# Attention of an attention, MoE and FFN kernel: two-step periods in a fixed order, the odd copies of transposed probabilities divided

## The reference

```python
batch, n_heads, seq, head_dim = (2, 8, 768, 64)
q_bits = (np.einsum('bhsd,dk->bhsk', q, proj) > 0)      # k_bits likewise
mask = q_bucket[:, :, :, None] == k_bucket[:, :, None, :]
scores = scale * np.matmul(q, k.transpose(0, 1, 3, 2))
scores = np.where(mask, scores, -1000000000.0)
scores = scores - np.max(scores, axis=-1, keepdims=True)
attn = np.exp(scores)
attn = attn / (np.sum(attn, axis=-1, keepdims=True) + 1e-09)
return np.matmul(attn, v)
```

## Time and profile before

| what | us |
|---|---|
| median of three runs | 1029.27 (1027.99 to 1030.33) |
| the profiled execution, its own time | 1037.7 |
| its span, first to last instruction | 1035.6 |
| TensorE busy in the span | 920.9 (89%) |
| VectorE, ScalarE, GpSimd busy | 428.7 (41%), 348.8 (34%), 416.7 (40%) |
| mean granted TensorE clock | 0.953 |

### The profile page before, as it was taken

The page is one execution under the profiler, slowest core; times in us unless marked ns, Lnnn a source line. Parts: engine busy times, 40 slices in busy tenths (PEclk is TensorE's granted clock), DMA queues, the critical chain, the costliest instruction groups (busy, mean ns, idle before and its releaser), DMA issues.

```text
span 1035.6 us, 15081 instructions
## 1 busy us (share of the span) xinstructions
PE 920.9 (89%) x4789; PEld 746.9 (72%) x4790; DVE 428.7 (41%) x756; ACT 348.8 (34%) x616; POOL 416.7 (40%) x247
## 2 busy tenths in 40 slices
PE   3699999999975389969999999999389999999998
PEld 3566666666643368858888888888279999999996
DVE  4567776677535812212222222222354333333222
ACT  1576677666734011111111111111223232323222
POOL 1222110000028585799594857689695001000000
PEclk8899999999998589989999999999789999999999
DMA  7444653356014279744352525245432011000000
GB/s 161 114 123 110 159 137 85 94 138 168 1 76 162 81 254 343 242 151 155 112 165 94 162 81 172 89 154 162 134 130 82 21 51 38 33 0 0 31 1 31
DMA packets 73237, 116.45 MB, mean 112 GB/s; under 512 B 31920, under 2 KB 33968, under 8 KB 73200
## 3 DMA queue, kind: packets, MB, share of 16 engines
q1 hardware_dynamic: 60592, 86.61, 28.0%
q0 software_dynamic: 4400, 14.42, 4.8%
q10 hardware_dynamic: 8208, 14.95, 4.4%
HBM read 73.49 MB, written 23.59 MB: 94 GB/s over the span
## 4 chain that ended last, share of the span: by engine, by line
PE 73%; DVE 7%; POOL 7%; DMA 6%; SPq 2%; issue 2%; ACT 2%; POOLq 0%; ACTq 0%; DVEq 0%
PE psS L726 13%; PE psT L683 12%; PE psS L667 11%; PE psS L741 9%; PE psV L565 6%; PE psT L554 4%; PE psV L741 4%; PE psS L543 4%; POOL W L433 3%; POOL W L431 2%; DMA x_sb<-x_dram,gather_i 2%; DVE W L796 2%; PE psS L692 2%; PE psM L530 2%; DMA staged<-in_moe_w 2%
## 5 line engine op out<-in xcount | busy, mean ns | idle before, releaser
L431 POOL TENSOR_TENSOR W<-staged,ones_col 128x1024 fp32r<-128x1024 f32 x80 | 152.7, 1909 | 167.9 <-DMA staged<-in_moe_w 103.8
L433 POOL TENSOR_TENSOR W<-staged,W 128x1024 fp32r<-128x1024 f32 x80 | 192.8, 2410 | 6.3
L667 PE MATMUL psS<-W,xT_hi 128*128 x448 | 144.4, 403 | 2.0 <-DVE xT_lo L969 2.0
L726 PE MATMUL psS<-x2T_hi,W 128*128 (+1 forms) x512 | 134.0, 343 | 1.6 <-DVE x2T_lo L987 1.6
L683 PE MATMUL psT<-W,hT_hi 128*128 x448 | 124.5, 410 | 9.2 <-POOL W L433 9.2
L802 DVE TENSOR_REDUCE neg_max<-psS 128x1 f32<-128x768 f32 x96 | 91.6, 954 | 48.9 <-PE psS L543 48.0
L1038 ACT ACTIVATE prob<-psS,exp_arg 128x768 f32<-128x768 f32 x96 | 95.5, 994 | 32.8 <-DVE exp_arg L805 32.7
L543 PE MATMUL psS<-W 128*128 128x384 f32 x384 | 93.4, 366 | 10.7 <-DMA W<-k_hi 9.3
L726 PEld LDWEIGHTS psS<-x2T_hi,W 128*128 128x128 f32 x512 | 94.5, 191 | 6.8 <-issue 2.0
L683 PEld LDWEIGHTS psT<-W,hT_hi 128*128 128x128 f32 x448 | 81.2, 191 | 24.7 <-issue 9.4
L1047 ACT ACTIVATE probT<-psT 128x768 f32<-128x768 f32 x96 | 78.1, 813 | 61.0 <-PE psT L554 59.5
(11 more groups left out here) (170 smaller groups left out, 1295.2 us busy)
## 6 DMA issues: line engine op xcount, KB each, us to landing
staged<-in_moe_w SPq DMA_DIRECT2D x64, 512.0 KB, 3.5
xs_dram<-x_sb SPq DMA_DIRECT2D x31, 256.0 KB, 4.8
x_in<-xs_dram ACTq DMA_DIRECT2D x29, 256.0 KB, 2.7
ys_dram<-y_sb ACTq DMA_DIRECT2D x28, 256.0 KB, 2.4
W<-q_hi SPq DMA_DIRECT2D x32, 192.0 KB, 3.4
W<-k_hi SPq DMA_DIRECT2D x32, 192.0 KB, 3.7
staged<-in_moe_w_in SPq DMA_DIRECT2D x8, 512.0 KB, 3.6
staged<-in_moe_w_out SPq DMA_DIRECT2D x8, 512.0 KB, 3.4
```

Source lines behind the costliest of these rows:

```text
L431: nc.gpsimd.tensor_tensor(W[:, at:at + CH], staged[:, n % 2], ones_col[:].to_broadcast([P, CH]), ALU.mult).then_inc(s_whi, 1)
L433: nc.gpsimd.tensor_tensor(W[:, at + BLOCK:at + BLOCK + CH], staged[:, n % 2], W[:, at:at + CH].bitcast(F32), ALU.subtract).then_inc(s_spli ...
L667: mm = nc.tensor.matmul(psS[:, 0, half], x[:, c * P:(c + 1) * P], W[:, bass.ds(slot + (w + c * F + half * 512), 512)], start=c == 0 and n ...
L726: mm = nc.tensor.matmul(psS[:, 0, f % 2, 0:GN], W[:, at:at + P], x[:, bass.ds(buf + c * GN, GN)], start=c == 0 and n == 0, stop=c == DC - ...
```

## The change

The TensorE order becomes a period of two steps (n even): T(n), unit of n, at t = 0 back, a part of W, T(n+1), S(n+3), unit of n+1, S(n+4). W moves from the odd step to between the two transposes, and at t = 0 the back and W part 0 are now in the same period. On VectorE the period is stats(n+2), collect, unit of n-1, normalise, unit of n, denominators, a new half copy for step n+1, stats(n+3). On odd steps ScalarE copies one bank of `psT` (384 columns) and VectorE the other (new semaphore `s_evD`). Units move: u0 to u3 of a pair run on the last four steps of the pair two before it (steps 8 to 11 of a pair), and u4 to u7 on steps 0, 2, 3 and 5. The first four units of pair 1 run ahead of T(0).

```diff
+        AHEAD = (-4, -3, -2, -1, 0, 2, 3, 5)
+
         def unit_at(n):
 
-            return n // PS + 1, n % PS
+            for pr in (n // PS + 1, n // PS + 2):
+                if pr < PAIRS and n - PS * (pr - 1) in AHEAD:
+                    return pr, AHEAD.index(n - PS * (pr - 1))
+            return None
...
             def transposes(n):
                 pe.wait_ge(s_exp, n + 1)
                 at_least(pe, s_evA, n)
+                at_least(pe, s_evD, n // 2)
...
                 if part == 0:
                     pe.wait_ge(s_evA, NT * (hd + 1))
+                    pe.wait_ge(s_evD, NT // 2 * (hd + 1))
...
-            for n in range(STEPS):
+            for n in range(-4, 0):
+                unit(*unit_at(n))
+            transposes(0)
+            scores(2)
+            for n in range(0, STEPS, 2):
                 hd, t = divmod(n, NT)
-                if n + 2 < STEPS:
-                    scores(n + 2)
-                transposes(n)
-                pr, u = unit_at(n)
-                if pr < PAIRS and u < UNITS:
-                    unit(pr, u)
+                if n:
+                    transposes(n)
+                if unit_at(n):
+                    unit(*unit_at(n))
                 if t == 0 and hd >= 2:
                     back(hd - 2)
-                if t % 2 and hd:
+                if hd:
                     weighted(hd - 1, t // 2)
+                transposes(n + 1)
+                if n + 3 < STEPS:
+                    scores(n + 3)
+                if unit_at(n + 1):
+                    unit(*unit_at(n + 1))
+                if n + 4 < STEPS:
+                    scores(n + 4)
...
+            def evac_half(n):
+
+                hd, t = divmod(n, NT)
+                dve.wait_ge(s_T, n + 1)
+                nc.vector.tensor_copy(probT[:, hd % 2, NT // 2:NT, t * P:(t + 1) * P],
+                                      psT[:, 1, 0:HALF].rearrange("p (c q) -> p c q", q=P)).then_inc(s_evD, 1)
+
...
-            for n in range(STEPS):
+            for n in range(-4, -1):
+                unit(*unit_at(n))
+            for n in range(0, STEPS, 2):
                 hd, t = divmod(n, NT)
+                if n + 2 < STEPS:
+                    statistics(n + 2)
                 if t == 0 and hd >= 2:
                     collect(hd - 2)
-                if t == 1 and hd >= 2:
+                if unit_at(n - 1):
+                    unit(*unit_at(n - 1))
+                if t == 0 and hd >= 2:
                     normalise(hd - 2)
-                if n:
-                    pr, u = unit_at(n - 1)
-                    if pr < PAIRS and u < UNITS:
-                        unit(pr, u)
-                if n + 2 < STEPS:
-                    statistics(n + 2)
+                if unit_at(n):
+                    unit(*unit_at(n))
                 if t == 2 and hd:
                     denominators(hd - 1)
+                evac_half(n + 1)
+                if n + 3 < STEPS:
+                    statistics(n + 3)
...
+                parts = 1 if n % 2 else 2
+                nc.scalar.activation(probT[:, hd % 2, 0:parts * (NT // 2), t * P:(t + 1) * P].rearrange("p (a c) q -> p a c q", a=parts),
+                                     psT[:, 0:parts, 0:HALF].rearrange("p a (c q) -> p a c q", q=P), ACT.Copy).then_inc(s_evA, 1)
...
             exponentials(0)
+            for n in range(-4, 0):
+                unit(*unit_at(n))
```

More of the change, by code:

```diff
@@ L233, in attention_moe_ffn @@
         s_evA = sem("s_evA")
+        s_evD = sem("s_evD")
         s_AV = sem("s_AV")
@@ L318, in attention_over @@
             eng.wait_ge(s_evA, STEPS)
+            eng.wait_ge(s_evD, STEPS // 2)
             eng.wait_ge(s_exp, STEPS)
@@ L1046, in evac @@
                     at_least(act, s_AV, CHUNKS * (hd - 1))
-                nc.scalar.activation(probT[:, hd % 2, :, t * P:(t + 1) * P].rearrange("p (a c) q -> p a c q", a=2),
-                                     psT[:, :, 0:HALF].rearrange("p a (c q) -> p a c q", q=P), ACT.Copy).then_inc(s_evA, 1)
+                parts = 1 if n % 2 else 2
+                nc.scalar.activation(probT[:, hd % 2, 0:parts * (NT // 2), t * P:(t + 1) * P].rearrange("p (a c) q -> p a c q", a=parts),
+                                     psT[:, 0:parts, 0:HALF].rearrange("p a (c q) -> p a c q", q=P), ACT.Copy).then_inc(s_evA, 1)
             for u in range(4):
@@ L1056, in _ @@
                 evac(n)
-                pr, u = unit_at(n)
-                if pr < PAIRS and u < 4:
-                    unit(pr, u)
+                if unit_at(n) and unit_at(n)[1] < 4:
+                    unit(*unit_at(n))
             attention_over(act)
```

## The result

The changed kernel takes 1076.57 us (median of four runs, 1073.72 to 1078.58) against 1029.8 us: 1.0447 of the time before, with a 95% interval of 1.0407 to 1.0486. It is slower by 46.8 us; the forecast was 1071 (1052 to 1097). Attention itself ends at 345.2 us instead of 304.5: +40.7, where the steps of the prediction gave +41.8. So the remainder varies by some 7 us from one execution to the next, that of before was a long one, and some 6 us between the two medians belong to no step that a trace shows.

A forecast was written before the change was run, and what follows sets the result against it. TensorE was taken as the bound, with a psT wait of 0.44 us per period. Terms 21.8 + 6.5 + 3.5 + 5.3 + 4.7 = +41.8 us, scaled to 41.5, gave 1029.3 + 41.5 = 1071 us (1052 to 1097).

The forecast's parts named there:

- the walk: Step-by-step timing of the new order through attention, period by period, from profiled durations; its terms sum to +41.8 us.
- The bare period: Two-step period without units or a head's start: 4.70 us instead of 4.86, a gain of 0.16.
- the loop through statistics, exponential and even copy: Bare period: S, statistics, exponential, copy, T, S close a loop of 4.70 us, whatever TensorE's own 4.29 is.
- A head's start: Period at t = 0: collect waits behind stats(n+2), W starts at 3.69 instead of about 1.1; 7.20 us without units.
- Units' waits: Periods with units: a unit waits for the previous unit's VectorE part behind stats(n+2); step 10 takes 6.4 us.
- A pair: Sum of a pair's six periods: 37.5 us against 33.9; over six pairs +21.8 us.
- The front: Start of attention: T(0) behind four units at 42.4 us, T(8) at 62.7 instead of 56.20: +6.5 us.
- GpSimd: Scaled q late for u0 of pairs 2 to 4: +3.5 us for pair 2, +5.3 for pairs 3 and 4.
- The clock: Rival: TensorE's granted clock falls at half the 14 head starts, 4 us each: +28, 1099 us; chance 0.12.
- my list of what would show the forecast wrong: Attention ending before 335 us, T(n+1) free at 2.2 us after T(n), or clock in attention below 1.00.
- tail: T(80) to the last head's W: 44.0 us against 39.2, given as +4.7 us.
- The case that was given 0.05: Rival: with collect and units' VectorE parts done before T(n), all waits go; 4.29 a period, about 1021 us; chance 0.05.

The follow-up runs named there:

- e1: Changed kernel, but at a head's start VectorE does collect and normalise (at step 0 also u3's subtraction) ahead of stats(n+2): 1050.59 us.
- e3: Changed kernel with VectorE doing collect, normalise and the units' parts ahead of stats(n+2) wherever they are waited for: 1043.71 us, 1.0124 of the kernel before.
- e8: Changed kernel with one more ScalarE copy of all 768 columns of psT, into a spare tile, ahead of each even copy: 1097.41 us.
- e4: Changed kernel with the divided odd copy undone, ScalarE copying all 768 columns on every step and VectorE none: 1077.91 us.
- e6: Changed kernel with collect, normalise and units ahead of stats(n+2), and GpSimd scaling the next pair's q before splitting this pair's weight chunk: 1028.34 us.
- e10: As e6, but back writes bank psM, W waits for collect alone, and back and normalise come later in the period: 1015.52 us.

## Why the prediction was right

**Sign and size.** Attention grew by 40.7 us where the steps gave 41.8, and e1 to e3 take the time back where the walk had put it, each within what was expected of it or 1 us beside. Point by point:

- **The bare period.** Forecast 4.70, measured 4.66 (before 4.85). That the loop through statistics, exponential and even copy closes it, and not TensorE, is shown by e8 (+0.70 for +0.70); that the divided odd copy brings nothing, by e4.
- **A head's start.** Forecast 7.20, 8.1 and 7.6; measured 7.09, 7.78 and 7.52. At the head's start without units the excess is VectorE's start of the next instruction 0.08 us behind the start of exp_arg, where I had it wait for the end, 0.16. Where the larger excess with u4 (8.1 against 7.78) lies was not followed up.
- **Units' waits.** Step 10 at 6.4, measured 6.33. A pair: 37.5 forecast, 36.8 measured.
- **The front.** Forecast +6.5, measured +11.1 (T(8) at 67.3). The order of events was right (T(0) at 42.4, measured 42.72), but two things behind it were missing. From T(0) to T(2) I walked with durations at the higher clock, 6.0 us where it took 8.7. With TensorE doing nothing but short transposes until 42.7, the clock stayed low: 0.62 on average from 20 to 60 us, and the first T took 1.49 us instead of 0.82. The other 1.9 us are at step 6, at the full clock: 6.06 us against the 4.2 of the walk, with exp_arg held by GpSimd's split. In e4, where the split's second instruction holds none and its first one for 0.8 us, that period is 4.32. (That step also has the first W in it, which the walk calls a period without W.)
- **GpSimd.** Forecast +8.8, measured at most 0.3: the page lists no such wait behind the front's. The term took 7.07 us from v's issue to the split from a place where four raw loads had just been issued ahead of v. Without them just ahead it is 4.52. Also T(8) came 4.6 us later than walked, which hid pair 2's wait; in e4, where T(8) is at 64.8, TensorE does wait 1.5 us for it. The mechanism is right all the same: it shows in e1 (3.35 us at step 32) as the forecast said it would with shorter periods, and goes in e6.
- **The clock,** a rival with 0.12, came in part: five falls of 1.5 us, 8 us, beside the forecast's mechanism and not in its place. I had priced one at 4 us. The falls are short, and part of each lies in a wait. A clock below 1.00 in attention was on my list of what would show the forecast wrong, and it came (0.92 to 0.96 in four of the windows); the other signs, an early end of attention and a free T(n+1) at 2.2 us, did not. By the rule of the Trainium skill named in the prediction ("TensorE: Matmul & The Clock Gate", "Why this matters for your kernels"), idle gaps between bursts cost clock. The trace agrees in part: all five falls stand behind gaps, of 0.74 to 1.56 us, but these are shorter than the gaps that the section warns of, equal ones at nine other starts cost nothing, and neither did one of 3.15 us in e1.

So the total is as close as it is because errors of both signs met: front and clock 12 us too low, GpSimd 8.5 and the periods and tail 5 too high. That is luck, in the total though not in the main term. (The tail's own difference is 44.0 - 39.2 = 4.8, not 4.7.) The remaining 5 to 6 us between 1071 and 1076.6 lie in the difference between the two medians that no trace of mine places.

**The case that was given 0.05,** TensorE alone setting the pace, has its condition met in e3 (collect ahead of the statistics) and still is 1043.7, not 1021. It was wrong that all waits would go. The closed loop of my own walk does not pass through collect, and it stays: the free period is 4.66 in e3, not 4.29. So does the trip through `psV`: 6.01 at a head's start. The front cost 8.9 us there (T(8) at 65.1), not 6.5, and GpSimd's q some 4, not 16. With GpSimd's order and the trip dealt with (e6, e10) it becomes 1015.5, and the loop is still there.

## What to carry to other kernels

In an order written out by hand, ask of each wait what stands ahead of the releasing instruction on its own engine: here collect stood behind a reduction that could only start when TensorE got to the very place where it then waited. A period that puts two users of one single-buffered bank next to each other exposes the whole trip through that bank, however short each part is. And before dividing a copy between engines, find out which of the copies closes the loop; the other one is free.

## What the runs showed of the hardware

- The granted TensorE clock fell inside attention although TensorE was 83 to 85% busy there (33.1 and 33.9 of 40 us). In after it fell at two heads' starts with waits of 1.06 and 1.54 us around a short back, at two with 1.55 and 0.74 around a unit and a back, and at one with 1.41 and 0.74; at nine starts with the same waits it did not. In e1, where these waits are shorter and TensorE was 84 and 88% busy in the same windows, it did not fall before T(95), although TensorE waited 1.61 and 3.15 us for q at steps 20 and 32; in e8 it fell in every period of step 6.
- A small instruction of VectorE with two inputs in SBUF (exp_arg, 128x2) can be held by GpSimd. In the traces of before, after and e6 it took over 0.3 us eleven times, up to 1.53 instead of 0.16, and each time it ended at most 0.03 us behind an instruction of GpSimd's split. The reductions and copies from PSUM beside them kept their length (neg_max 0.94 at 62.64 us). No run took the split away to test it.
- A reduction on VectorE starts 0.08 us after the start of the small operation ahead of it (304.37 to 304.45), so this one costs less than its 0.16 us in a chain.
- S directly behind S, a price that no row of before had, is 0.71: the eight matmuls of two S in a row last 1.66 us in after (302.39), and one S 0.95.
